# A fused attention, mixer and expert kernel: q and k laid out before launch, two score passes per head, and a weight split moved from the attention to the mixer

## What is computed

```python
scores = scale * q @ k.T
bias = -slopes[head] * dist
keep = is_global | is_local
a = softmax(where(keep, scores + bias, -1e9))
x = a @ v
h = x.T @ U @ V
u = x + h.T
x = u + relu(u @ w_ch1) @ w_ch2
out[s] = p[e] * relu(x[s] @ w1[e]) @ w2[e]
```

## Time and profile before

| what | value |
|---|---|
| median of 3 runs | 690.82 us (686.25 to 690.89) |
| span of the profiled execution, first to last instruction | 689.6 us |
| share of PE (matmul) busy | 90% |
| share of DVE, ACT, POOL busy | 45%, 37%, 14% |
| granted TensorE clock, mean over the span | 0.965 |

### The profile page before, as it was taken

One profiled execution on the slowest core, in us unless ns is written; L12 is line 12 of the kernel. 1 busy time (PEld: TensorE's weight loads), 2 busy tenths in 40 slices (PEclk: granted clock), 3 DMA queues, 4 the chain that ended last, 5 costly groups with the idle time before them and its releaser, 6 DMA issues.

```text
span 689.6 us, 11540 instructions
## 1 busy us (share of the span) xinstructions
PE 621.2 (90%) x3430; PEld 541.6 (79%) x3431; DVE 308.2 (45%) x670; ACT 254.1 (37%) x554; POOL 96.6 (14%) x145
## 2 busy tenths in 40 slices
PE   0899899989999999999999999925899998999994
PEld 0789889938999998989998999824677876887883
DVE  5688888624332212220222011483665447574521
ACT  1677788613221111111111201321655346464411
POOL 6634433000000000000000000001112111212111
PEclk9999999999999999999999999955999999999998
DMA  8965676001111100010001000234684528654310
GB/s 209 201 151 118 135 150 142 1 0 62 61 62 62 47 0 1 1 46 1 1 1 46 1 1 1 72 126 151 209 284 155 185 70 284 242 200 159 115 43 21
DMA packets 72175, 65.78 MB, mean 95 GB/s; under 512 B 53807, under 2 KB 53807, under 8 KB 72144
## 3 DMA queue, kind: packets, MB, share of 16 engines
q1 hardware_dynamic: 64800, 50.87, 25.3%
...
q10 hardware_dynamic: 3024, 0.61, 0.6%
...
...
## 4 chain that ended last, share of the span: by engine, by line
PE 82%; DVE 6%; issue 4%; DMA 3%; ACT 2%; SPq 1%; DVEq 0%; POOL 0%; ACTq 0%; POOLq 0%
PE bank L452 65%; PE bank L900 3%; PE bank L1173 2%; PE bank L1190 2%; PE bank L496 2%; PE bank L1156 2%; DMA raw<-in_moe_w_dram 2%; PE bank L1189 2%; ACT hs L955 1%; DVE q_parts L1339 1%; PE bank L515 1%; PE bank L524 1%; DVE wbuf L595 1%; PE bank L844 1%; DMA limits<-in_n_local_dram 1%
## 5 line engine op out<-in xcount | busy, mean ns | idle before, releaser
L452 PE MATMUL bank<-uT,wbuf 128*128 128x384 f32 x768 | 144.8, 336 | 1.5 <-DVE uT L670 1.5
L452 PE MATMUL bank<-wbuf,hid 128*128 128x512 f32 x576 | 145.1, 396 | 0.0
L452 PEld LDWEIGHTS bank<-uT,wbuf 128*128 128x128 f32 x768 | 136.2, 188 | 7.0 <-issue 1.7
L703 DVE SCALAR_TENSOR_TENSOR hid<-bank,hid 128x384 fp32r<-128x384 f32 x64 | 35.7, 557 | 214.9 <-ACT hid L644 214.9
L452 PEld LDWEIGHTS bank<-wbuf,hid 128*128 128x128 f32 x576 | 106.0, 188 | 20.6 <-issue 0.7
L644 ACT ACTIVATE hid<-bank 128x384 fp32r<-128x384 f32 x64 | 31.5, 492 | 230.0 <-PE bank L452 230.0
L595 DVE TENSOR_TENSOR wbuf<-raw,wbuf 128x1024 fp32r<-128x1024 f32 x72 | 85.1, 1221 | 27.3 <-ACT wbuf L591 26.5
L452 PE MATMUL bank<-wbuf,xT 128*128 128x512 f32 x360 | 93.1, 410 | 1.7 <-DVE xT L985 1.7
L591 ACT CAST wbuf<-raw 128x1024 fp32r<-128x1024 f32 x72 | 72.9, 1047 | 41.4 <-PE bank L452 20.4
L452 PE MATMUL bank<-wbuf,hT 128*128 128x512 f32 x360 | 86.0, 394 | 0.0
L452 PEld LDWEIGHTS bank<-wbuf,xT 128*128 128x128 f32 x360 | 69.6, 197 | 16.3 <-issue 2.1
...
## 6 DMA issues: line engine op xcount, KB each, us to landing
raw<-in_moe_w_dram SPq DMA_DIRECT2D x64, 512.0 KB, 4.1
raw<-in_moe_w_ch_dram POOLq DMA_DIRECT2D x12, 512.0 KB, 5.9
...
raw<-in_moe_w_ch_dram SPq DMA_DIRECT2D x4, 512.0 KB, 3.5
...
```

The source lines that it names most:

```text
L452: last = pe.matmul(dst, lhs[a], rhs[b_], start=start and i == 0, stop=stop and i == 2)
L703: dve.scalar_tensor_tensor(hid[i % 2][:, 1, :], bank[3 + i % 2][:, 0:BN], 0.0, hid[i % 2][:, 0, :].bitcast(F32), ALU.max, ALU.subtract).th ...
```

## The change

**Layout on the host.** q and k come transposed and with their 64 rows twice, `[pair, 128, head, S]`; v comes with a column of ones behind each head's 64 and with its windows copied out, so one transfer of 128x1430 brings a pair's values; `w_ch1` comes in units of 256 columns; U, V, the gates and the limits are laid out as they are used. Nothing is added or multiplied on the host.

**Two passes.** Of q, rows 64 to 127 hold hi and rows 0 to 63 hold lo; of k all 128 rows hold hi in one matrix and lo in a second. A contraction over 128 rows then gives (lo + hi) times k's hi, and a second one times k's lo. The unit of work is now a group `g`, both heads of a tile (48 groups). The keys are no longer copied into windows, so for `t > 0` each pass is two matmuls, one over 32 and one over 224 columns, all with one stationary operand. PE does scores of `g`, turn of `g-2`, weigh of `g-3`. The hardware loop is unrolled.

**Sums.** The column of ones gives the row sums in the output matmul (65 columns in place of 64); ACT no longer sums. DVE adds 1e-9, inverts and multiplies (`normalise`).

**Who splits q and k.** ACT copies hi of q (`split_q`, 128x1536), DVE hi of k (`split_k`, 128x1536), POOL subtracts both lo parts (`split_qk`, 64x1536 and 128x1536) for the next pair. POOL no longer clears `q_parts` and no longer splits `w_ch1`. It makes eight biases once, two in each of the first four pairs; they are used for both batches.

**Weights.** The 16 units of `w_ch1` and `w_ch2` form one list, `ENTRIES`. Four are loaded in the attention and split by ACT and DVE at the mixer's start, one before the first block, eleven in it.

The core of the diff:

```diff
+        ENTRIES = [(0, i) for i in range(RAW)]
+        for i in range(RAW):
+            ENTRIES += [(1, i), (0, RAW + i)]
+        ENTRIES += [(1, i) for i in range(RAW, UNITS)]
+        def load_raw(sp, k):
+            which, i = ENTRIES[k]
+            sp.dma_start(raw[:, k % RAW, :], (w_ch1, w_ch2)[which][i, :, :]).then_inc(raw_in[k % RAW], 16)
...
+                    if kb == 0:
+                        pe.wait_ge(lo_split, entry_of(0, f // 2) + 1)
                     for c in range(DC):
-                        cols_f = slice(c * FF + f * P, c * FF + (f + 1) * P)
+                        at = f // 2 * UNIT + c * COLS + f % 2 * P
+                        cols_f = slice(at, at + P)
...
+        def entry_hi(act, k):
+            which, i = ENTRIES[k]
+            act.wait_ge(raw_in[k % RAW], 16 * (k // RAW + 1))
+            act.copy(wbuf[which][:, 0, i, :], raw[:, k % RAW, :]).then_inc(hi_split, 1)
+        def entry_lo(dve, k):
+            which, i = ENTRIES[k]
+            w = wbuf[which]
+            dve.wait_ge(hi_split, k + 1)
+            dve.tensor_tensor(w[:, 1, i, :], raw[:, k % RAW, :], w[:, 0, i, :].bitcast(F32),
+                              ALU.subtract).then_inc(lo_split, 1)
+        def entries_after(f):
+            if f < 2 * RAW:
+                return [RAW + 1 + f]
+            return [2 * RAW + (f + 1) // 2] if f % 2 and f < NF - 1 else []
...
             act.copy(v_parts[:, :], v_raw[:, :]).then_inc(v_hi, 1)
+            for k in range(RAW):
+                entry_hi(act, k)
...
-                    if kb == 0 and f % 2 and f // 2 + 1 < UNITS:
-                        split(f // 2 + 1)
+                    if kb == 0:
+                        for k in entries_after(f):
+                            entry_hi(act, k)
...
+            def load_qk(n):
+                cols_n = slice(WIN if n == 0 else 0, S)
+                sp.dma_start(k_raw[n % 2][:, :, cols_n], kT[n, :, :, cols_n]).then_inc(qk_in[n % 2], 16)
+                sp.dma_start(q_raw[n % 2][:, :, cols_n], qT[n, :, :, cols_n]).then_inc(qk_in[n % 2], 16)
+            def load_v(n):
+                sp.dma_start(vs[n % 2][:, :], vw[n, :, :]).then_inc(v_in[n % 2], 16)
+            sp.dma_start(q_raw[0][:, :, 0:WIN], qT[0, :, :, 0:WIN]).then_inc(qk_first, 16)
+            sp.dma_start(k_raw[0][:, :, 0:WIN], kT[0, :, :, 0:WIN]).then_inc(qk_first, 16)
+            load_qk(0)
+            load_v(0)
+            load_qk(1)
+            sp.dma_start(u_sb[:, :, :, :], moe_U).then_inc(const_in, 16)
+            sp.dma_start(v_raw[:, :], moe_V).then_inc(const_in, 16)
             with sp.If(path(sp)):
-                pairs(sp, load_pair)
+                for n in range(PAIRS):
+                    if n + 1 < PAIRS:
+                        late_enough(sp, pv_done, TB * n)
+                        load_v(n + 1)
+                    if n + 2 < PAIRS:
+                        if n == 0:
+                            sp.wait_ge(lo_first, 3)
+                        sp.wait_ge(parts, 2 * n + 1)
+                        load_qk(n + 2)
+                    if n % 2:
+                        load_raw(sp, n // 2)
...
+            for k in range(RAW, 2 * UNITS):
+                sp.wait_ge(lo_split, k - RAW + 1)
+                load_raw(sp, k)
...
-            def turn_qk(n, par, j):
-                src, loaded = ((qs, q_in), (ks, k_in))[j // 2]
-                if j % 2 == 0:
-                    wait_loop(pe, loaded, 32 * (n + 1))
-                wait_loop(pe, tr_dve, BATCHES * n + j + 1)
-                for i in range(HALF):
-                    last = pe.transpose(tr_bank[j % 2][:, i * P:(i + 1) * P],
-                                        src[:, HALF * (j % 2) + i, :, :].rearrange("p h d -> p (h d)"), ident[:, :])
-                last.then_inc(tr_done, 1)
...
-                passes(pe, dst[:, 0:width(s)], [q_parts[:, par, a, h, t * P:(t + 1) * P] for a in range(2)],
-                       [k_parts[:, par, a, t, WIN - width(s):WIN] for a in range(2)], True, True).then_inc(qk_done, 1)
...
+            def scores(g):
+                n, t = divmod(g, TB)
+                par = n % 2
+                if t == 0:
+                    if n == 0:
+                        pe.wait_ge(lo_first, 2)
+                    else:
+                        pe.wait_ge(parts, 2 * n + 1)
+                if g == 2:
+                    pe.wait_ge(lo_first, 3)
+                    pe.wait_ge(parts, 1)
+                late_enough(pe, scored, 2 * g - 2)
+                spans = ((0, slice(0, P)),) if t == 0 else ((0, slice(0, GLOB)), (GLOB, slice((t - 1) * P + GLOB, (t + 1) * P)))
+                for h in range(2):
+                    for a in range(2):
+                        for at, keys in spans:
+                            dst = score_bank[2 * (g % 2) + h][:, at:at + keys.stop - keys.start]
+                            last = pe.matmul(dst, q_parts[:, par, h, t * P:(t + 1) * P], k_parts[:, par, a, h, keys],
+                                             start=a == 0 and at == 0, stop=a == 1, skip_group_check=True)
+                last.then_inc(qk_done, 1)
...
+                for h in range(2):
+                    pe.wait_ge(exped, 2 * g + h + 1)
+                    for c in range(width(t) // P):
+                        at = h * WIN + c * P
+                        last = pe.transpose(turn_bank[g % 2][:, at:at + P], PR[g % 3][:, h, c * P:(c + 1) * P], ident[:, :])
...
+            def weigh(g):
+                n, t = divmod(g, TB)
+                par, half = n % 2, t // HALF
+                pe.wait_ge(*((pt_dve, dve_copies(g)) if copied_by_dve(t) else (pt_act, act_copies(g))))
                 if t == 0:
+                    pe.wait_ge(v_in[par], 16 * (n // 2 + 1))
+                if t % HALF == 0:
+                    late_enough(pe, normed, 2 * (n - 1) + half + 1)
+                for h in range(2):
+                    at = (t % HALF) * VW + h * (D + 1)
+                    dst = out_bank[half][:, at:at + D + 1]
+                    def values(i):
+                        return vs[par][:, i * VW + h * (D + 1):i * VW + (h + 1) * (D + 1)]
+                    if t == 0:
+                        last = pe.matmul(dst, PT[g % 3][:, h, 0:P], values(0), start=True, stop=True)
+                    else:
+                        pe.matmul(dst, PT[g % 3][:, h, 0:P], values(TB + t - 1), start=True, stop=False)
+                        last = pe.matmul(dst, PT[g % 3][:, h, P:WIN], values(t), start=False, stop=True)
...
+                for g in range(GROUPS + WEIGH_LAG):
+                    if g < GROUPS:
+                        scores(g)
+                    if 0 <= g - TURN_LAG < GROUPS:
+                        turn_probs(g - TURN_LAG)
+                    if g >= WEIGH_LAG:
+                        weigh(g - WEIGH_LAG)
...
+            act.wait_ge(qk_in[0], 32)
+            act.copy(q_parts[:, 0, :, WIN:S], q_raw[0][:, :, WIN:S]).then_inc(hi_first, 1)
+            act.copy(k_parts[:, 0, 0, :, WIN:S], k_raw[0][:, :, WIN:S]).then_inc(hi_first, 1)
+            def split_q(n):
+                act.wait_ge(qk_in[n % 2], 32 * (n // 2 + 1))
+                late_enough(act, qk_done, TB * (n - 1))
+                act.copy(q_parts[:, n % 2, :, :], q_raw[n % 2][:, :, :]).then_inc(q_hi, 1)
...
+                for g in range(GROUPS + TURN_LAG):
+                    if g >= TURN_LAG:
+                        keep_turned(g - TURN_LAG)
+                    if g < GROUPS:
+                        exponentials(g)
+                        if g % TB == 0 and g // TB + 1 < PAIRS:
+                            split_q(g // TB + 1)
...
+            def split_k(n):
+                dve.wait_ge(qk_in[n % 2], 32 * (n // 2 + 1))
+                late_enough(dve, qk_done, TB * (n - 1))
+                dve.tensor_copy(k_parts[:, n % 2, 0, :, :], k_raw[n % 2][:, :, :]).then_inc(k_hi, 1)
...
+            def keep_turned(g):
+                t = g % TB
+                if not copied_by_dve(t):
+                    return
+                dve.wait_ge(turned, g + 1)
+                late_enough(dve, pv_done, g - 2)
+                dve.tensor_copy(PT[g % 3][:, :, :].rearrange("p h n -> p (h n)"), turn_bank[g % 2][:, :]).then_inc(pt_dve, 1)
...
+                dve.tensor_scalar(each, of[:, :, :, D:D + 1], 1.0e-9, None, ALU.add).then_inc(inv_step, 1)
+                dve.wait_ge(inv_step, at + 1)
+                dve.reciprocal(inv[:, :], inv[:, :]).then_inc(inv_step, 1)
...
+                for g in range(GROUPS + HALF + 2):
+                    if g < GROUPS:
+                        score(g)
+                        if g % TB == 1 and g // TB + 1 < PAIRS:
+                            split_k(g // TB + 1)
+                    if 0 <= g - TURN_LAG < GROUPS:
+                        keep_turned(g - TURN_LAG)
+                    if g >= TB and g % HALF == 0 and g - WEIGH_LAG < GROUPS:
+                        normalise(*divmod((g - TB) // HALF, 2))
```

(24 more changed lines are left out.)

618 lines of the change are left out of this document (217 added, 401 removed).

## The result

The changed kernel takes **751.35 us** (median of 4 runs, 746.16 to 754.11) against 690.68 us before (4 runs, 686.25 to 690.89). The ratio is 1.089, its 95% interval 1.083 to 1.095. I had predicted 671 us, in a range of 658 to 686. The change is slower, by nearly 9%.

A forecast was written before the change was run, and what follows sets the result against it. PE was taken to set the attention's pace; pairs of 12.5 us would start its mixer 19.8 us earlier, so 689.6 - 19.8 = 669.8 us of span, plus 1.2 for the median: 671 us, range 658 to 686.

The forecast's parts named there:

- So 11.66 us: PE's work per attention pair: scores 5.28, transposes of probabilities 2.42 and passes with v 3.96 us.
- The second pass saved is spent on the cut at column 32: PE's scores: eight matmuls of 32 and 224 columns take 0.96 us a group, against 0.90 now.
- 19.8 us gain: End of the attention: PE's mixer starts at 118.5 us and not at 138.3.
- A pair: Attention: 12.5 us a pair after the change against 14.46 now, bounds 11.7 (PE alone) and 14.5 (nothing gained).
- wait of 0.65: PE, each pair: it wants the turned probabilities at 4.96 us and has them at 5.6, giving 12.3 a pair.
- two other loops at 12.0 to 12.3: Attention: POOL's subtractions let the next pair start at 12.3 us; transfers with POOL and ACT end at 12.0.
- mis-sized term: PE's passes with v: 0.72 us a group, 3.96 a pair, the 65th column costing nothing the rows can show.
- The start: Attention's beginning: loads, splits and biases let pair 1 begin at 25.7 us.
- rival C: Attention: reciprocal caught by POOL's subtractions, or transfers at 210 GB/s and not 318; pairs of 14.4, 682 us; chance 0.14.
- Rival E: Mixer: the moved weight splits lie on the path after all, up to 9.8 us more, 681 us; chance 0.06.
- Rival B: Attention: POOL's subtraction beats DVE's copy of k to their shared port; pairs of 16.2, 692 to 693 us; chance 0.15.
- signs of being wrong: DVE's copy losing the race in most pairs, 32-column matmuls far from 0.1 us, or PE awaiting a split in the mixer.

The follow-up runs named there:

- e2: The change without the cut at column 32, one 256-column matmul per pass, leaving out the global keys of tiles 2 to 5: 660.7 us, one run.
- e7: The kernel before with its three score passes each cut at column 32, layout, transfers and row sums untouched: 809.2 us, one run.
- e1: The change plus 14 filler score matmuls of 512 columns in PE's idle stretch before the third score group: 666.66, 668.19, 750.95 and 748.06 us.
- e8: The change plus 14 filler matmuls of 512 columns ahead of group 24, the first of the fifth pair: 707.81 us, one run.
- e11: The change plus 14 filler matmuls of 512 columns in front of the fourth score group: median 673.19 us, 0.977 of the kernel before.
- e9: The change plus ten early ones matmuls and 32 fillers of 512 columns before the third score group: 667.18, 668.18, 667.21 and 751.76 us.
- e6: e5 with score tile t = 1 in one uncut span of 256 columns: 751.34, 662.0, 735.5 and 738.01 us.
- e5: The change plus ten early ones matmuls and 18 fillers of 512 columns before the third score group: 750.6, 745.6, 669.12, 753.2, 749.14 and 751.99 us.

## Why the prediction was wrong, step by step

**The step that failed** is the price of PE's work, "So 11.66 us" a pair, and under it a premise that no sentence stated: that each matmul of the changed kernel would take the spacing of the earlier trace rows, which are rows at the upper level. The count of instructions was right, but not the level at which they ran. The working even took the cut for a matter of 0.06 us a group ("The second pass saved is spent on the cut at column 32"); e2 and e7 show that the cut keeps the level down, and e1, e8 and e11 that the level decides between 12.4 and 23.25 us a pair. Over the attention that is the 61.1 us lost at the mixer's start and the 19.8 us gain that never came. No rival had it: each changed a wait, a transfer or the price of a narrow matmul, none the level.

The sign was in the rows. In the earlier trace rows PE's first six 128-column matmuls of the kernel before span 1.61 us. In the earlier trace rows three take 0.53, so six would take 0.53 + 3 x 0.12 = 0.89. The first scores of the kernel before run at the lower level, beside a row that reads 1.00, and the earlier trace rows have 0.91 for the stage behind the attention's last wait. The question "what brings it up between 21 and 28 us, and is that still there after the change?" was not asked. (The clock's first record in that trace is a rise at 26.39 us.)

**With the level up the rest of the prediction holds** (e1, e11):

- A pair: 12.5 us predicted, 12.38 in e1 and 41.84 - 29.49 = 12.35 in e11. But not for the reason given; that 12.5 came out so near is luck. PE is busy for 75.00 of 75.00 us there, so the 12.35 are its own work: the "wait of 0.65" and the two other loops at 12.0 to 12.3 do not show. The mis-sized term is v: 33.46 - 32.65 = 0.81 us a group and not 0.72, in e11's whole pair 4.54 and not 3.96. Scores (0.97, predicted 0.96) and transposes (0.43, predicted 0.44) were right. A sum too small by 0.7 met a wait that was not there: in e11 the turned probabilities are out 5.18 us after the pair's first scores (5.6 predicted), and PE starts on them at 5.23 (4.96 predicted; its 1.66 for the second group's start is a slip, the terms add up to 1.64).
- The start: pair 1 at 25.7 predicted, 24.91 in e1. PE's mixer at 118.5 predicted, 116.82 in e1, 121.37 in e11 with its 5 us of fillers.
- DVE's copy of k: 0.95 predicted, 0.956 in e1. The reciprocal stayed at 0.19, so rival C's first half did not happen; its second half, slower transfers, would show as a wait of PE, and from 25 to 100 us e11 has none.
- The rest behind the attention: 551 predicted, 549.3 measured. Rival E did not happen.
- The time: 671 predicted. e1 and e9 have 666.7 to 668.2 where they come up.
- POOL's subtraction of 1536 columns: 3.6 predicted, 3.43 to 3.46 where it waits for nothing.

**Rival B's mechanism is real but cost little here.** The groups of DVE's copy of k, in the change as it stands and in e1 (both from 24 to 116 us):

```profile
L1317 DVE CAST k_parts<-k_raw 128x1536 fp32r<-128x1536 f32 x4 | 11.1, 2785 | 0.0
```

```profile
L1321 DVE CAST k_parts<-k_raw 128x1536 fp32r<-128x1536 f32 x6 | 5.7, 956 | 0.0
```

One of the prediction's own signs of being wrong came true with it: six of the seven copies in the change lost the race. With PE at the lower level the order of events shifts and POOL's subtraction begins first (at 34.20 and 57.44, the copies at 35.67 and 58.91), so the copy is held to 2.8 us; PE, never idle, does not notice. With PE at the upper level DVE won each time in e1, e8, e9 and e11. In e1's second pair:

```profile
28.54 0.96 DVE L1321 CAST k_parts<-k_raw 128x1536 fp32r<-128x1536 f32 x1
...
28.68 4.13 POOL L1406 TENSOR_TENSOR q_parts<-q_raw,q_parts 64x1536 fp32r<-64x1536 f32 x1 [2.26 <-ACT q_parts L1241]
```

DVE is 0.14 us ahead (0.2 predicted: as close as feared), and now it is POOL that is held: 4.13 us and not 3.44. In e8 both orders stand in one trace: after the first copy, the next three, at the lower level, take 2.78 to 2.81 us, the last three, at the upper, 0.96. So TensorE's speed decides the race. In e6 the lost race did cost something, each time an idle stretch with which the level went.

**What stays open.** Why a matmul stream with pieces of 32 and 224 columns does not raise the level and uncut 256 columns do was not taken apart further: the width, the number of weight loads and the number of matmuls change together in e2 and e7, while the columns stay the same. Nor is it only the cut scores that can be too little: behind them PE does transposes and passes with v alone, and the level came up there in the change (195.56 us) and not in e5. Why e1, e5, e6 and e9 come up in some executions and not in others is open; what happened is shown only for the profiled ones; the run of 751.76 of e9 has no profile. A layout that gives each tile its 256 keys in one piece, so that the cut goes and the result stays, was not built. e2 shows about what it could reach, 660.7 us, without the copies that it would need.
